# Attention, routed experts and a feed-forward layer on one core: main rows of seven experts 624 instead of 640

## The chip, the cores and the metric

The kernel runs on one core of one Trainium2 chip. The metric is the device time of one execution in microseconds (us), and the time of a kernel is the median of several executions. Engines are named as in the profile: PE (TensorE, its matmuls), PEld (TensorE's weight loads, which overlap the matmuls), DVE (VectorE), ACT (ScalarE), POOL (GpSimd) and SP (SyncE, which here only issues DMAs).

## The reference

Three layers, one after the other, all in fp32, on 4 x 576 = 2304 tokens of width 512:

```python
# 1. attention with a sliding window of 64 keys, 8 heads of 64
mask = (rel >= 0) & (rel < 64)
x = softmax(where(mask, q @ k.T / 8, -1e9)) @ v          # [2304, 512]
# 2. eight experts, the two best of each token
noisy = x @ w_gate + log1p(exp(x @ w_noise)) * noise      # [2304, 8]
top2, top2_w = two largest of noisy, softmax over the two
out[mask] += top2_w[mask, k, None] * (np.maximum(x[mask] @ w1[e], 0.0) @ w2[e])
# 3. feed-forward layer
h = x @ w_in;  g = h * np.clip(h + 3.0, 0.0, 6.0) / 6.0
out = g @ w_out
```

`w1[e]` is 512 x 1024 and `w2[e]` is 1024 x 512; `w_in` is 512 x 2048 and `w_out` 2048 x 512. Each token goes to two of the eight experts, so an expert gets 2 x 2304 / 8 = 576 rows on average. Counted with the reference on its own inputs, the experts 0 to 7 take 618, 582, 571, 549, 537, 554, 611 and 586 rows, and expert 0 has 377 of its rows in the first 11 of the 18 token tiles.

## The kernel before

**Stages.** Attention runs over 18 tiles of 128 tokens (`iteration`). Each tile's result also goes through the gate, and in five lots of tiles DVE works out which two experts a token has and which place it takes among the expert's rows. POOL then scatters each token's row twice into `x_sorted` in DRAM (`scatter`, L691), at `e * ROOM + rank`. Then come the eight experts (`expert`, one after the other), then the feed-forward layer over six groups of three tiles (`hidden2` L1706, `project2` L1722), whose rows POOL gathers from `y_sorted`.

**An expert.** The first MAIN = 640 rows of expert e are always worked, as BLOCKS = 5 blocks of 128 rows in two parts, PARTS = ((0, 3), (3, 2)): part 0 is blocks 0 to 2 (384 rows), part 1 is blocks 3 and 4 (256 rows). A block of x is loaded from `x_sorted` into `x_in` (`load_x`, an ACT DMA), transposed by four PE operations (`turn_x`, L1570), and split by ACT and DVE into a high and a low half (`x_hi` L868, `x_lo` L1167) that stand in `xs`. All matmuls are done as three passes over such halves. For each chunk c of 128 of the 1024 hidden features, `hidden` (L1586) does 4 x 3 = 12 matmuls with the weights as the loaded side and the part's rows as the streamed side: 384 columns in part 0, 256 in part 1. ACT takes the relu of the result (`h_hi`, L878), DVE makes the low half (`h_lo`, L1173). Then `project` (L1602) does, for each block of the part, three matmuls with the block's 128 hidden rows as the loaded side and 512 columns of `w2` streamed, into the block's bank of `Y`. After the last chunk, DVE moves each block to `y_sb` (`move_y`, L1185) and ACT stores it to `y_sorted` (`store_y`, L888). PE's order is written out by hand: hidden(0), hidden(1), project(0), hidden(2), project(1) and so on, with the transposes of coming blocks put between (TURN_AT): blocks 3 and 4 of the same expert in part 0, blocks 0 to 2 of the next expert in part 1. So `project(c)` follows a whole `hidden(c + 1)` after `hidden(c)`.

**Rows beyond the main ones.** Where an expert has more rows than MAIN, `tab_live` is set (L1226), and all engines run `more_block` MORE times (13, each 128 rows), with a wait of its own at each step. Otherwise they skip it.

**Places.** Expert e's rows begin in `y_sorted` at the sum of its predecessors' row counts, each rounded up to whole blocks of 128. Stores of the five blocks are issued in order of the experts, and `store_y` of block 0 waits until all of the expert before are stored. Since part 0 of expert 0 begins when only the first 11 tiles are scattered, the count of expert 0 is raised to at least PARTS[0][1] * P = 384 at that point (L1117), and its rows that no token takes are zeros.

**Expert 0 and the start of expert 1.** The rank of the last lot is worked out while part 0 of expert 0 runs (`rank`, between `hidden(3)` and `project(2)`). From it follow, in this order: eight scatters on POOL, SP's loads of blocks 3 and 4 of expert 0 (L570), SP's writing of zeros behind the rows of expert 1 (`pad`, L556), and ACT's loads of expert 1's first blocks, which `turn_x` in part 1 of expert 0 waits for.

**Weights.** SP loads them in eight chunks an expert into `stage`; POOL splits each into halves (L660, L670) into one of two sets of `W`, which it may overwrite when the expert before the last one is done (`expert_done`).

Of the kernel before, what the change touches and what calls it, by code (L numbers as in the profile page):

```python
# [5 lines left out]
ALU = mybir.AluOpType  # L6
ACT = mybir.ActivationFunctionType
AX = mybir.AxisListType
F32 = mybir.dt.float32
# [8 lines left out]
def attention_moe_ffn(nc, q, k, v, wg, wn, noise, w1, w2, w_in, w_out, out):  # L18
# [23 lines left out]
    assert MAIN + MORE * P == N  # L42
# [16 lines left out]
    assert GT * P <= PARTS[0][1] * P  # L59
# [46 lines left out]
    ROOM = N + MAIN  # L106
# [96 lines left out]
    ex = Region((nc.sbuf_usable_end - 64 - 4 * (3 * DM + DM + F + 2 * F + (3 + BLOCKS) * DM + 2 * KD * MAIN)) // 128 * 128 + 64)  # L203
# [27 lines left out]
    with ExitStack() as ctx:  # L231
# [92 lines left out]
        y_stored = [sem(f"y_stored{j}") for j in range(BLOCKS)]  # L324

# [118 lines left out]
        def x_place(j, a):  # L444

            part = 0 if j < PARTS[1][0] else 1
            at = (j - PARTS[part][0]) * P
            return xs[part][:, a, :, at:at + P]
# [13 lines left out]
        def _(sp):  # L462
# [106 lines left out]
            for j in range(PARTS[1][0], BLOCKS):  # L569
                sp.dma_start(x_in[:, j], x_sorted[j * P:(j + 1) * P, :]).then_inc(x_loaded[j], 16)  # L570
# [24 lines left out]
        def _(pool):  # L595
# [197 lines left out]
        def _(act):  # L793
# [46 lines left out]
            def load_x(e, j):  # L840
                row = e * ROOM + j * P
                src = x_sorted[row:row + P, :] if isinstance(e, int) else x_sorted[bass.ds(row, P), :]
                act.dma_start(x_in[:, j], src).then_inc(x_loaded[j], 16)
# [22 lines left out]
            def x_hi(e, j, bank=XTP):  # L866
                act.wait_ge(tx_full, BLOCKS * e + j + 1)
                nc.scalar.copy(x_place(j, 0), bank.rearrange("p (k n) -> p k n", k=KD)).then_inc(xhi_done, 1)  # L868
# [26 lines left out]
            def more_block(e, t):  # L895
# [14 lines left out]
                act.wait_ge(more_moved, o + 2)  # L910
                act.dma_start(y_sorted[bass.ds(row_y, P), :], y_more[:]).then_inc(more_stored, 16)
# [97 lines left out]
        def _(dve):  # L1009
# [5 lines left out]
            for j in range(BLOCKS):  # L1015
                dve.sem_inc(y_stored[j], 16)
            dve.sem_inc(more_xlo, 1)
# [54 lines left out]
            def route(b, part):  # L1072
# [37 lines left out]
                elif part == 5:  # L1110
# [6 lines left out]
                    if b == FIRST_LOT:  # L1117
                        step(nc.vector.tensor_scalar(base_e[:, 0:1], base_e[:, 0:1], float(PARTS[0][1] * P), None, ALU.max))
# [46 lines left out]
            def x_lo(e, j, bank=XTP):  # L1165
                dve.wait_ge(xhi_done, BLOCKS * e + j + 1)
                nc.vector.tensor_tensor(x_place(j, 1), bank.rearrange("p (k n) -> p k n", k=KD),  # L1167
                                        x_place(j, 0).bitcast(F32), ALU.subtract).then_inc(x_split, 1)

            def h_lo(e, part, c):  # L1170
                n = PARTS[part][1] * P
                dve.wait_ge(hhi_done, unit(e, part, c) + 1)
                nc.vector.scalar_tensor_tensor(hs[:, c % 2, 1, 0:n], HP_[:, c % 2, 0:n], 0.0,  # L1173
                                               hs[:, c % 2, 0, 0:n].bitcast(F32), ALU.max, ALU.subtract).then_inc(h_split, 1)

            def move_y(e, j):
# [8 lines left out]
                nc.vector.tensor_copy(y_sb[:, j % 3], Y[:, j, :]).then_inc(y_moved, 1)  # L1185
# [166 lines left out]
        def _(pe):  # L1352
# [212 lines left out]
            def turn_x(e, j, bank=XTP):  # L1565
                pe.wait_ge(x_loaded[j], 16 * (e + 1))
                if bank is XTP:
                    pe.wait_ge(x_split, BLOCKS * e + j + 1)
                for kd in range(KD):
# [21 lines left out]
            def project(e, par, part, c):  # L1591
# [182 lines left out]
```

## Time and profile before

| what | us |
|---|---|
| median of 3 runs | 1024.81 |
| lowest and highest of them | 1022.99, 1029.31 |
| the profiled execution, its own time | 1028.99 |
| its span, first to last instruction | 1027.2 |
| PE busy in the span | 996.3 |
| PEld, POOL, DVE, ACT busy | 885.0, 423.6, 416.9, 229.6 |

The span is what all positions in time in the trace are counted from. A matmul's duration in the trace is the time from its start to its modelled end, and neighbours overlap, so 12 matmuls in a row take less than 12 times the mean duration of one. The rows on the chain of waits don't overlap, and give the pace. The mean granted clock of TensorE over the span is 0.990 of full speed.

### The profile page before, as it was taken

Reading aid. Unit: us, or ns where it says so; the run is one execution under the profiler, and the core shown is the slowest. Engines: PE = TensorE matmul, PEld = TensorE weight load, DVE = VectorE, ACT = ScalarE, POOL = GpSimd, SP = SyncE. Lnnn points to the kernel's source line nnn. Section 1 sums busy time; section 2 is a strip of 40 time slices with the busy share of each in tenths; the row PEclk is TensorE's granted clock in tenths of the full one; section 3 lists DMA queues with packets and bytes.
Section 4 is the critical chain, followed back from the end, with each engine's and each line's share of the span. In section 5 each row is a group of like instructions: output and inputs, shape, how many; then the busy total and the mean of one; then the engine's idle time right before and its main releaser. Section 6 shows DMA issues by size and latency. Waiting matters only on the chain.

```text
span 1027.2 us, 17992 instructions
## 1 busy us (share of the span) xinstructions
PE 996.3 (97%) x7108; PEld 885.0 (86%) x7108; DVE 416.9 (41%) x897; ACT 229.6 (22%) x537; POOL 423.6 (41%) x326
## 2 busy tenths in 40 slices
PE   6998879999999999999999999999999999999998
PEld 5776668898999999999989988999999999999997
DVE  3577754313222221322222246545435445454433
ACT  4665621211111121111111122111111111111111
POOL 3167885994664819194663928300101001000000
PEclk9999989999999999999999999999999999999999
DMA  9699786855362616254341334110101011100000
GB/s 183 133 198 238 219 274 216 259 178 181 104 215 77 200 64 218 80 155 163 103 164 66 120 119 157 49 45 21 42 31 41 21 45 39 39 1 1 32 1 32
DMA packets 125542, 116.17 MB, mean 113 GB/s; under 512 B 64800, under 2 KB 92960, under 8 KB 125472
## 3 DMA queue, kind: packets, MB, share of 16 engines
q1 hardware_dynamic: 106368, 75.36, 26.3%
q10 hardware_dynamic: 13344, 20.98, 5.9%
q0 software_dynamic: 5760, 18.88, 5.6%
q8 instruction: 47, 0.77, 0.3%
q14 instruction: 23, 0.19, 0.1%
HBM read 76.13 MB, written 39.06 MB: 112 GB/s over the span
## 4 chain that ended last, share of the span: by engine, by line
PE 87%; POOL 4%; DVE 3%; DMA 2%; issue 2%; ACT 1%; SPq 1%; ACTq 0%; DVEq 0%; POOLq 0%
PE PS L1602 20%; PE PS L1586 20%; PE PS L1722 19%; PE PS L1706 19%; POOL x_sorted L691 2%; PE PS L1467 2%; PE PS L1570 2%; PE PS L1391 1%; PE PS L1446 1%; POOL W L670 1%; PE PS L1647 1%; PE PS L1430 1%; DMA x_sorted<-zeros 1%; DVE negmax L1038 1%; POOL W L660 1%
## 5 line engine op out<-in xcount | busy, mean ns | idle before, releaser
L1602 PE MATMUL PS<-W,hs_room 128*128 128x512 f32 x960 | 245.6, 399 | 0.0
L1586 PE MATMUL PS<-xs,W 128*128 128x256 f32 (+1 forms) x1536 | 243.7, 309 | 0.0
L1586 PEld LDWEIGHTS PS<-xs,W 128*128 128x128 f32 x1536 | 234.3, 189 | 10.4 <-issue 0.2
L1722 PE MATMUL PS<-W,gs 128*128 128x512 f32 x864 | 217.0, 395 | 0.9 <-DVE gs L1322 0.9
L1706 PE MATMUL PS<-x2s,W 128*128 128x384 f32 x1152 | 216.6, 337 | 0.0
L1706 PEld LDWEIGHTS PS<-x2s,W 128*128 128x128 f32 x1152 | 201.2, 188 | 7.3
L660 POOL TENSOR_TENSOR W<-stage,ones_f 128x1024 fp32r<-128x1024 f32 (+1 forms) x100 | 147.5, 1483 | 141.3 <-PE PS L1602 137.5
L1602 PEld LDWEIGHTS PS<-W,hs_room 128*128 128x128 f32 x960 | 174.6, 188 | 33.2
L1722 PEld LDWEIGHTS PS<-W,gs 128*128 128x128 f32 x864 | 161.2, 188 | 31.8 <-issue 1.6
L670 POOL TENSOR_TENSOR W<-stage,W 128x1024 fp32r<-128x1024 f32 (+1 forms) x100 | 185.6, 1865 | 5.9
L1173 DVE SCALAR_TENSOR_TENSOR hs_room<-PS,hs_room 128x256 fp32r<-128x256 f32 (+1 forms) x128 | 62.8, 491 | 294.1 <-ACT hs_room L878 294.1
L878 ACT ACTIVATE hs_room<-PS 128x256 fp32r<-128x256 f32 (+1 forms) x128 | 56.0, 438 | 374.6 <-PE PS L1586 356.8
L983 ACT ACTIVATE gs<-PS 128x384 fp32r<-128x384 f32 x96 | 47.2, 492 | 307.6 <-DVE PS L1320 307.6
L767 POOL DMA_INDIRECT ya<-y_sorted,slot x18 | 17.1, 951 | 224.0 <-PE PS L1647 200.7
L1318 DVE TENSOR_SCALAR hc<-PS 128x384 f32<-128x384 f32 x96 | 53.5, 557 | 130.9 <-PE PS L1706 130.9
L1322 DVE SCALAR_TENSOR_TENSOR gs<-PS,gs 128x384 fp32r<-128x384 f32 x96 | 53.6, 558 | 60.5 <-ACT gs L983 60.0
L1320 DVE SCALAR_TENSOR_TENSOR PS<-hc,PS 128x384 f32<-128x384 f32 x96 | 53.9, 562 | 3.3
L691 POOL DMA_INDIRECT x_sorted<-x_cur,slot_cur x36 | 35.8, 994 | 19.1 <-DVE slot_cur L1124 11.9
L813 ACT ACTIVATE probs<-PS,negmax 128x128 f32<-128x128 f32 x144 | 39.3, 399 | 2.9 <-DVE negmax L1038 2.9
L1185 DVE COPY y_sb<-PS 128x512 f32<-128x512 f32 x40 | 27.0, 688 | 22.5 <-PE PS L1602 22.4
L1167 DVE TENSOR_TENSOR xs<-PS,xs 128x512 fp32r<-128x512 f32 x40 | 27.6, 691 | 18.6 <-ACT xs L868 16.9
L698 POOL COPY x_cur<-x_new 128x512 f32<-128x512 f32 x18 | 10.9, 609 | 50.6 <-DVE x_new L1053 50.4
(133 smaller groups left out, 576.9 us busy)
## 6 DMA issues: line engine op xcount, KB each, us to landing
stage<-in_moe_w_dram SPq DMA_DIRECT2D x64, 512.0 KB, 5.6
y_sorted<-y_sb ACTq DMA_DIRECT2D x40, 256.0 KB, 3.0
x_in<-x_sorted ACTq DMA_DIRECT2D x38, 256.0 KB, 4.5
x_sorted<-zeros SPq DMA_DIRECT2D x7, 1280.0 KB, 7.8
vD<-in_v_dram SPq DMA_DIRECT2D x72, 64.0 KB, 3.0
out_dram<-o_sb SPq DMA_DIRECT2D x18, 256.0 KB, 2.0
stage<-in_moe_w_in_dram SPq DMA_DIRECT2D x8, 512.0 KB, 3.9
stage<-in_moe_w_out_dram SPq DMA_DIRECT2D x8, 512.0 KB, 3.4
```

Source lines behind the costliest of these rows:

```text
L660: last = nc.gpsimd.tensor_tensor(chunk_at(parity, c, 0)[:, at], stage[:, c % STAGES, at], ones_f[:].broadcast_to([P, n]), ALU.mult)
L670: last = nc.gpsimd.tensor_tensor(chunk_at(parity, c, 1)[:, at], stage[:, c % STAGES, at], chunk_at(parity, c, 0)[:, at].bitcast(F32), ALU. ...
L691: pool.indirect_dma_start(out=x_sorted, out_offset=bass.IndirectOffsetOnAxis(ap=slot_cur[:, k, t:t + 1], axis=0), in_=x_cur[:, t, :], in_o ...
L878: nc.scalar.activation(hs[:, c % 2, 0, 0:n], HP_[:, c % 2, 0:n], ACT.Relu).then_inc(hhi_done, 1)
L1173: nc.vector.scalar_tensor_tensor(hs[:, c % 2, 1, 0:n], HP_[:, c % 2, 0:n], 0.0, hs[:, c % 2, 0, 0:n].bitcast(F32), ALU.max, ALU.subtract). ...
L1318: nc.vector.tensor_scalar(hc[:, c % 2], h, 3.0, 0.0, ALU.add, ALU.max).then_inc(hc_done, 1)
L1320: nc.vector.scalar_tensor_tensor(G6[:, c % 2], hc[:, c % 2], 6.0, h, ALU.min, ALU.mult).then_inc(g6_done, 1)
L1322: nc.vector.scalar_tensor_tensor(gs[:, c % 2, 1], G6[:, c % 2], 1.0 / 6.0, gs[:, c % 2, 0].bitcast(F32), ALU.mult, ALU.subtract).then_inc( ...
L1586: last = nc.tensor.matmul(HP_[:, c % 2, 0:n], W[:, par, 0, b, at:at + P], xs[part][:, a, kd, :], start=start, stop=(kd == KD - 1 and (a, b ...
L1602: last = nc.tensor.matmul(Y[:, first + t, :], hs[:, c % 2, a, t * P:(t + 1) * P], W[:, par, 1, b, c * DM:(c + 1) * DM], start=(c == 0 and ...
L1706: last = nc.tensor.matmul(H2P[:, c % 2, :], W[:, 0, kd // 2, b, at:at + P], x2s[par][:, a, kd, :], start=first, stop=(kd == KD - 1 and (a, ...
L1722: last = nc.tensor.matmul(OP[:, tt, :], gs[:, c % 2, a, tt * P:(tt + 1) * P], W[:, 1, c // FC, b, at:at + DM], start=(c == 0 and (a, b) == ...
```

## The change

For experts 0 to 6 block 2, the last of part 0, has 112 rows instead of 128. Part 0 thus has 368 rows, part 1 still 256, and MAIN is 624. Blocks 3 and 4 begin 16 rows earlier in `x_sorted` and `y_sorted`. Expert 7 keeps its 640 rows in `E - 1`'s own code, since `is_last` is true for it. The 16 rows of `y_sorted` behind the 624 are filled with zeros by a small DMA of ACT's queue for each of the seven experts (64 pieces of 512 bytes, in `store_y` after block 0), with a semaphore `y_filled` on which the next expert's block 0, `more_block`'s store and POOL's gathers wait. MORE becomes 14. The count of expert 0 is raised to 368 instead of 384.

The core of the diff:

```diff
-    MAIN = BLOCKS * P
-    MORE = (N - MAIN) // P
+    CUT = 16
+    MAIN = BLOCKS * P - CUT
+    MORE = -(-(N - MAIN) // P)
...
+    def block_rows(e, j):
+        return P - CUT if j == PARTS[0][1] - 1 and not is_last(e) else P
+
+    def block_row(e, j):
+
+        return j * P - (CUT if j >= PARTS[0][1] and not is_last(e) else 0)
...
             for j in range(PARTS[1][0], BLOCKS):
-                sp.dma_start(x_in[:, j], x_sorted[j * P:(j + 1) * P, :]).then_inc(x_loaded[j], 16)
+                sp.dma_start(x_in[:, j], x_sorted[block_row(0, j):block_row(0, j) + P, :]).then_inc(x_loaded[j], 16)
...
+            pool.wait_ge(y_filled, 16 * E)
...
-                act.dma_start(x_in[:, j], src).then_inc(x_loaded[j], 16)
+                act.dma_start(x_in[0:n, j], src).then_inc(x_loaded[j], 16)
...
             def h_hi(e, part, c):
-                n = PARTS[part][1] * P
+                n = part_rows(e, part)
...
                         act.wait_ge(y_stored[n], 16 * (e + 1))
+                    act.wait_ge(y_filled, 16 * (e + 1))
                     act.wait_ge(more_stored, 16 * (MORE * e + 1))
                 act.wait_ge(y_moved, BLOCKS * (e + 1) + j + 1)
-                act.dma_start(y_sorted[bass.ds(base + j * P, P), :], y_sb[:, j % 3]).then_inc(y_stored[j], 16)
+                n = block_rows(e, j)
+                act.dma_start(y_sorted[bass.ds(base + block_row(e, j), n), :], y_sb[0:n, j % 3]).then_inc(y_stored[j], 16)
+                if j == 0 and not is_last(e):
+
+                    act.dma_start(y_sorted[bass.ds(base + MAIN, CUT), :].rearrange("p (k d) -> (p k) d", d=P),
+                                  zeros[0:CUT * KD, :]).then_inc(y_filled, 16)
...
-                        step(nc.vector.tensor_scalar(base_e[:, 0:1], base_e[:, 0:1], float(PARTS[0][1] * P), None, ALU.max))
+                        step(nc.vector.tensor_scalar(base_e[:, 0:1], base_e[:, 0:1], float(part_rows(0, 0)), None, ALU.max))
...
-                nc.vector.tensor_copy(y_sb[:, j % 3], Y[:, j, :]).then_inc(y_moved, 1)
+                n = block_rows(e, j)
+                nc.vector.tensor_copy(y_sb[0:n, j % 3], Y[0:n, j, :]).then_inc(y_moved, 1)
...
-                    last = nc.tensor.transpose(bank[:, kd * P:(kd + 1) * P], x_in[:, j, kd * P:(kd + 1) * P], ident[:])
+                    last = nc.tensor.transpose(bank[:, kd * P:kd * P + n], x_in[0:n, j, kd * P:(kd + 1) * P], ident[0:n, 0:n])
...
             def hidden(e, par, part, c):
-                n = blocks * P
+                n = part_rows(e, part)
...
-                        last = nc.tensor.matmul(HP_[:, c % 2, 0:n], W[:, par, 0, b, at:at + P], xs[part][:, a, kd, :],
+                        last = nc.tensor.matmul(HP_[:, c % 2, 0:n], W[:, par, 0, b, at:at + P], xs[part][:, a, kd, 0:n],
...
                 for t in range(blocks):
+                    n = block_rows(e, first + t)
                     for a, b in PASSES:
-                        last = nc.tensor.matmul(Y[:, first + t, :], hs[:, c % 2, a, t * P:(t + 1) * P],
+                        last = nc.tensor.matmul(Y[0:n, first + t, :], hs[:, c % 2, a, t * P:t * P + n],
```

PE's order of work stays as it was, with other sizes. This is PE at the end of part 0 of expert 1 in the kernel before; `xs_116` is part 0's `xs` and `xs_115` part 1's, and the sizes are those of the result:

```order
L1586 MATMUL PS<-xs_116,W 128x384 x12
L1570 MATMUL PS<-ident,x_in 128x128 x4
L1602 MATMUL PS<-W,hs_room 128x512 x9
L1586 MATMUL PS<-xs_116,W 128x384 x12
L1602 MATMUL PS<-W,hs_room 128x512 x18
L1654 TENSOR_LOAD tab_live
L1654 ISA x2
L1586 MATMUL PS<-xs_115,W 128x256 x24
```

And the same place in the changed kernel, whose lines are numbered 32 and 33 higher here:

```order
L1618 MATMUL PS<-xs_116,W 128x368 x12
L1602 MATMUL PS<-ident,x_in 128x128 x4
L1635 MATMUL PS<-W,hs_room 128x512 x6
L1635 MATMUL PS<-W,hs_room 112x512 x3
L1618 MATMUL PS<-xs_116,W 128x368 x12
L1635 MATMUL PS<-W,hs_room 128x512 x6
L1635 MATMUL PS<-W,hs_room 112x512 x3
L1635 MATMUL PS<-W,hs_room 128x512 x6
L1635 MATMUL PS<-W,hs_room 112x512 x3
L1687 TENSOR_LOAD tab_live
L1687 ISA x2
L1618 MATMUL PS<-xs_115,W 128x256 x24
```

Nothing moved; each of the 12 matmuls of a chunk streams 368 columns, and of nine matmuls of `project` three load 112 columns and write 112 partitions.

This is ACT at the start of part 1 of expert 1 before:

```order
L878 ACTIVATE hs_room<-PS 128x256
L888 ISA
L888 DMA y_sorted<-y_sb 128x512
L888 ISA
L888 DMA y_sorted<-y_sb 128x512
L878 ACTIVATE hs_room<-PS 128x256
L888 ISA
L888 DMA y_sorted<-y_sb 128x512
```

And in the changed kernel:

```order
L899 ACTIVATE hs_room<-PS 128x256
L911 ISA
L911 DMA y_sorted<-y_sb 128x512
L914 ISA
L914 DMA y_sorted<-zeros 64x128
L911 ISA
L911 DMA y_sorted<-y_sb 128x512
L899 ACTIVATE hs_room<-PS 128x256
L911 ISA
L911 DMA y_sorted<-y_sb 112x512
```

One DMA more stands between the relu of chunk 0 and that of chunk 1, and the store of block 2 carries 112 rows.

## Rows read from the trace of the kernel before

**Rows 1.** The page: busy time of the engines; the chain that ended last.

```profile
PE 996.3 (97%) x7108; PEld 885.0 (86%) x7108; DVE 416.9 (41%) x897; ACT 229.6 (22%) x537; POOL 423.6 (41%) x326
...
PE 87%; POOL 4%; DVE 3%; DMA 2%; issue 2%; ACT 1%; SPq 1%; ACTq 0%; DVEq 0%; POOLq 0%
```

**Rows 2.** Stretches (from:to, length in us): expert 0's parts, then expert 4's.

```profile
core 0: us, PE busy (x) PEld busy (x) DVE busy (x) ACT busy (x) POOL busy (x), PEclk, DMA share, GB/s
144.50:181.40 36.90, 36.90 (x197) 32.99 (x196) 17.05 (x78) 6.14 (x14) 21.18 (x20) 0.96 0.76 255
...
380.10:414.40 34.30, 34.30 (x177) 31.02 (x176) 7.74 (x14) 5.00 (x10) 33.22 (x16) 1.00 0.63 200
414.40:438.20 23.80, 23.80 (x157) 21.60 (x156) 6.63 (x14) 4.76 (x11) 0.84 (x1) 1.00 0.17 56
```

**Rows 3.** The chain in order of time through expert 4: start us, length us, what.

```profile
380.28 4.17 PE PS L1586 x24
384.45 2.10 PE PS L1602 x9
...
405.79 0.44 PE PS L1570 x4
...
410.41 4.19 PE PS L1602 x18
```

**Rows 4.** The same chain, part 1.

```profile
414.60 2.83 PE PS L1586 x24
417.43 1.40 PE PS L1602 x6
```

**Rows 5.** Groups of instructions, shapes apart, 380.1 to 438.2 us: busy, mean ns, idle before.

```profile
L1586 PEld LDWEIGHTS PS<-xs,W 128*128 128x128 f32 x192 | 29.1, 188 | 1.3
L1602 PEld LDWEIGHTS PS<-W,hs_room 128*128 128x128 f32 x120 | 21.8, 188 | 4.2
...
L660 POOL TENSOR_TENSOR W<-stage,ones_f 128x1024 fp32r<-128x1024 f32 x8 | 15.2, 1894 | 23.5 <-PE PS L1602 23.5
...
L1173 DVE SCALAR_TENSOR_TENSOR hs_room<-PS,hs_room 128x384 fp32r<-128x384 f32 x8 | 4.5, 557 | 23.5 <-ACT hs_room L878 23.5
...
L878 ACT ACTIVATE hs_room<-PS 128x384 fp32r<-128x384 f32 x8 | 3.9, 492 | 26.7 <-PE PS L1586 26.7
```

**Rows 6.** Instructions in order of time, start of part 1 of expert 4: start, length in us.

```profile
416.71 0.97 ACTq L888 DMA_DIRECT2D y_sorted<-y_sb  x2
...
417.85 0.38 ACT L878 ACTIVATE hs_room<-PS 128x256 fp32r<-128x256 f32 x1 [1.32 <-DVE y_sb L1185]
...
418.26 0.42 DVE L1173 SCALAR_TENSOR_TENSOR hs_room<-PS,hs_room 128x256 fp32r<-128x256 f32 x1 [0.68 <-ACT hs_room L878]
...
420.44 0.94 PE L1602 MATMUL PS<-W,hs_room 128*128 128x512 f32 x3
```

**Rows 7.** The chain in order of time, from the last scatters into part 1 of expert 0.

```profile
162.46 0.95 POOL x_sorted L691
...
171.44 2.72 DMA x_sorted<-x_cur,slot_cur
...
175.89 7.38 DMA x_sorted<-zeros
...
183.29 4.07 DMA x_in<-x_sorted
...
187.40 0.65 PE PS L1570 x4
```

**Rows 8.** Instructions in order of time around the start of expert 0 and its rank.

```profile
143.12 0.58 ACT L868 CAST xs<-PS 128x512 fp32r<-128x512 f32 x1 [1.05 <-PE PS L1570]
...
143.74 0.69 DVE L1167 TENSOR_TENSOR xs<-PS,xs 128x512 fp32r<-128x512 f32 x1 [0.20 <-ACT xs L868]
...
144.53 3.71 PE L1586 MATMUL PS<-xs,W 128*128 128x384 f32 x12
...
159.31 0.19 PE L1509 MATMUL PS<-chosen_b,before_b 128*128 128x32 bf16 x1
```

More of the change, by code:

```diff
@@ L36, in attention_moe_ffn, with is_last, part_rows @@
     BLOCKS = 5
-    MAIN = BLOCKS * P
-    MORE = (N - MAIN) // P
+    CUT = 16
+    MAIN = BLOCKS * P - CUT
+    MORE = -(-(N - MAIN) // P)
     FEWEST = -(-2 * N // P)
     MOST = (2 * N + PARTS[0][1] * P + E * (P - 1)) // P + BLOCKS
-    assert MAIN + MORE * P == N
+    def is_last(e):
+        return isinstance(e, int) and e == E - 1
+    def block_rows(e, j):
+        return P - CUT if j == PARTS[0][1] - 1 and not is_last(e) else P
+    def block_row(e, j):
+        return j * P - (CUT if j >= PARTS[0][1] and not is_last(e) else 0)
+    def part_rows(e, part):
+        first, blocks = PARTS[part]
+        return sum(block_rows(e, j) for j in range(first, first + blocks))
+    assert all(sum(part_rows(e, part) for part in range(2)) >= MAIN for e in range(E)) and MAIN + MORE * P >= N
     FC = F // P
@@ L58, in attention_moe_ffn @@
     MIX_AT = {4: (0, 1), 5: (2,)}
-    assert GT * P <= PARTS[0][1] * P
+    assert GT * P <= part_rows(E - 1, 0)
     assert KD * F == QCH * CH and KD * F2 == SCH * CH and FC * DM == QCH * CH and F2C * DM == SCH * CH
@@ L104, in attention_moe_ffn @@
     assert LOTS[0][0] + LOTS[0][1] + RANKS_AFTER - 1 == LOOP[0] + LOOP_TILES and LOTS[0][1] == most - 1
-    ROOM = N + MAIN
+    ROOM = N + BLOCKS * P
     x_sorted = nc.dram_tensor("x_sorted", [E * ROOM, DM], F32).ap()
@@ L198, in attention_moe_ffn @@
     assert late.at <= nc.sbuf_usable_end
-    ex = Region((nc.sbuf_usable_end - 64 - 4 * (3 * DM + DM + F + 2 * F + (3 + BLOCKS) * DM + 2 * KD * MAIN)) // 128 * 128 + 64)
+    ex = Region((nc.sbuf_usable_end - 64 - 4 * (3 * DM + DM + F + 2 * F + (3 + BLOCKS) * DM + 2 * KD * BLOCKS * P)) // 128 * 128 + 64)
     assert base % 128 == 0
@@ L324, in attention_moe_ffn @@
         y_stored = [sem(f"y_stored{j}") for j in range(BLOCKS)]
+        y_filled = sem("y_filled")
         more_loaded = sem("more_loaded")
@@ L442, in if_more, with x_place, x_turned @@
                     eng.sem_inc(signal, each * MORE)
-        def x_place(j, a):
+        def x_place(e, j, a):
             part = 0 if j < PARTS[1][0] else 1
             at = (j - PARTS[part][0]) * P
-            return xs[part][:, a, :, at:at + P]
+            return xs[part][:, a, :, at:at + block_rows(e, j)]
+        def x_turned(e, j, bank):
+            return bank.rearrange("p (k n) -> p k n", k=KD)[:, :, 0:block_rows(e, j)]
         def unit(e, part, c):
@@ L840, in load_x @@
             def load_x(e, j):
-                row = e * ROOM + j * P
-                src = x_sorted[row:row + P, :] if isinstance(e, int) else x_sorted[bass.ds(row, P), :]
-                act.dma_start(x_in[:, j], src).then_inc(x_loaded[j], 16)
+                row, n = e * ROOM + block_row(e, j), block_rows(e, j)
+                src = x_sorted[row:row + n, :] if isinstance(e, int) else x_sorted[bass.ds(row, n), :]
+                act.dma_start(x_in[0:n, j], src).then_inc(x_loaded[j], 16)
             for T in range(TILES + 1):
@@ L867, in x_hi @@
                 act.wait_ge(tx_full, BLOCKS * e + j + 1)
-                nc.scalar.copy(x_place(j, 0), bank.rearrange("p (k n) -> p k n", k=KD)).then_inc(xhi_done, 1)
+                nc.scalar.copy(x_place(e, j, 0), x_turned(e, j, bank)).then_inc(xhi_done, 1)
             def h_hi(e, part, c):
-                n = PARTS[part][1] * P
+                n = part_rows(e, part)
                 act.wait_ge(h_full, unit(e, part, c) + 1)
@@ L910, in more_block @@
                 act.wait_ge(more_moved, o + 2)
+                if not is_last(e):
+                    act.wait_ge(y_filled, 16 * (e + 2))
                 act.dma_start(y_sorted[bass.ds(row_y, P), :], y_more[:]).then_inc(more_stored, 16)
@@ L1016, in _ @@
                 dve.sem_inc(y_stored[j], 16)
+            dve.sem_inc(y_filled, 16)
             dve.sem_inc(more_xlo, 1)
@@ L1166, in x_lo @@
                 dve.wait_ge(xhi_done, BLOCKS * e + j + 1)
-                nc.vector.tensor_tensor(x_place(j, 1), bank.rearrange("p (k n) -> p k n", k=KD),
-                                        x_place(j, 0).bitcast(F32), ALU.subtract).then_inc(x_split, 1)
+                nc.vector.tensor_tensor(x_place(e, j, 1), x_turned(e, j, bank), x_place(e, j, 0).bitcast(F32), ALU.subtract)\
+                    .then_inc(x_split, 1)
             def h_lo(e, part, c):
-                n = PARTS[part][1] * P
+                n = part_rows(e, part)
                 dve.wait_ge(hhi_done, unit(e, part, c) + 1)
@@ L1568, in turn_x @@
                     pe.wait_ge(x_split, BLOCKS * e + j + 1)
+                n = block_rows(e, j)
                 for kd in range(KD):
-                    last = nc.tensor.transpose(bank[:, kd * P:(kd + 1) * P], x_in[:, j, kd * P:(kd + 1) * P], ident[:])
+                    last = nc.tensor.transpose(bank[:, kd * P:kd * P + n], x_in[0:n, j, kd * P:(kd + 1) * P], ident[0:n, 0:n])
                 last.then_inc(tx_full, 1)
@@ L1575, in hidden @@
                 first, blocks = PARTS[part]
-                n = blocks * P
+                n = part_rows(e, part)
                 if c == 0:
```

## The prediction

> **What bounds the kernel now.** I read the page's busy times first: PE is busy 97% of the span, and 87% of the chain that ended last is PE [rows 1]. A share over the whole kernel doesn't say what an edit in the experts is worth, so next comes the table of stretches: in expert 4, which stands for experts 1 to 6, PE is busy 34.30 of 34.30 us in part 0 and 23.80 of 23.80 us in part 1, at a granted clock of 1.00 [rows 2], which is the 2.4 GHz level. No other engine is near that. The chain in order of time shows the pace, since its pieces don't overlap: in part 0, 24 matmuls of `hidden` in 4.17 us, or 173.8 ns each for 384 columns, and 9 of `project` in 2.10 us, or 233.3 ns each for 512 columns [rows 3]; in part 1, 24 of `hidden` in 2.83 us, or 117.9 ns each for 256 columns [rows 4]. The reader is to see that time follows the streamed columns: 0.452, 0.456 and 0.461 ns a column for 384, 512 and 256. A fixed cost per matmul would make the small ones much dearer by column. The loads of the other operand, 188 ns each as recorded [rows 5], lie beneath the matmuls; matmuls with a load each still follow each other at 117.9 ns.
>
> The other engines leave slack. POOL splits the next weights in some 33 us of part 0 [rows 2] and then sits idle 23.5 us until PE frees a set [rows 5]. ACT's relu (492 ns) and DVE's low half (557 ns) make 1.05 us behind a `hidden` of 384 columns [rows 5], and a whole further `hidden` of about 2.08 us lies before the `project` that needs them. So a shorter stream on PE should come out in the time, one for one, until such a cover is gone.
>
> **The change, part by part.**
>
> *Shorter `hidden`, experts 1 to 6.* Each has 8 x 12 = 96 matmuls in part 0 that lose 16 columns. The slope between the two sizes of the same line is (173.8 - 117.9) / 128 = 0.436 ns a column [rows 3, 4], so 16 columns are 7.0 ns. In all 6 x 96 x 7.0 ns = 4.02 us. Bounds: by the mean cost of a column, 0.452 ns, it is 4.17 us; below, nothing, if 368 columns ran like 384. No row shows a length between 256 and 384, and 368 is no multiple of 64, but three sizes lie within 2% of one line, so I take the slope.
>
> The Trainium skill, page "TensorE: Matmul & The Clock Gate", section "Back-to-back issue gap", gives N / 2.4 + 2.5 ns for one matmul after another. By it 384 columns would take 162.5 ns, and the rows show 173.8; the saving of 16 columns would be 6.7 ns, and this term 3.84 us instead of 4.02. The measured slope stands in the sum.
>
> *Expert 0.* The same 96 matmuls, but the first 12 run at the lower pace: 12 in 3.71 us from the first start to the modelled end of the last [rows 8], with the granted clock at 0.96 over the stretch [rows 2]. As an estimate, 3.71 us / 12 x 16 / 384 = 12.9 ns each, 0.15 us. The other 84 give 84 x 7.0 = 0.59 us. Together 0.74 us earlier at the end of part 0. But this expert has a second chain. PE's transposes of expert 1's first block wait for a load that began at 183.29 us, behind the zeros that began at 175.89, behind scatters that began at 162.46, and the transposes start at 187.40 when it lands [rows 7]. That chain starts from the last rank on PE at 159.31 [rows 8], which stands behind four of eight chunks of `hidden`: it comes earlier by 12 x 12.9 + 36 x 7.0 ns = 0.41 us, while PE comes earlier by 0.74 us. PE already waits there, so 0.33 us is lost in a longer wait. Net 0.41 us.
>
> *Shorter transposes.* Block 2's four transposes take 0.44 us as 110 ns each [rows 3] for 128 streamed columns. With 112 they could be 110 x 16 / 128 = 13.8 ns shorter, if the stream sets the pace, or not at all, if the load does; nothing in the rows tells these apart, since both are 128. Six times four in the stream make 0 to 0.33 us; I take 0.15, near the middle.
>
> *Start of expert 0.* Block 2 is the last thing before the first `hidden`: ACT 0.58 us, then DVE 0.69 us, ending at 144.43, and PE starts at 144.53 [rows 8]. With an eighth less each and shorter transposes this chain would be 0.16 to 0.2 us shorter, but PE's own work before it leaves room for only part. I take 0.1, between 0 and 0.2.
>
> *`project`.* The 7 x 8 x 3 = 168 matmuls of block 2 still stream 512 columns, so they stay at 233.3 ns [rows 3]. Fewer loaded columns and fewer result rows save nothing where the stream sets the pace. Cost and gain 0.
>
> *The added zeros.* ACT issues one DMA more, between two stores, in part 1. Two such issues take 0.97 us, so one costs about 0.49 us [rows 6]. Behind it on ACT stand the store of block 1 and the relu of chunk 1, which started at 417.85 and whose low half was ready at 418.68; PE uses it at 420.44 [rows 6]. So 1.76 us of cover hides 0.49 us, the cover being `project` of chunk 0 and `hidden` of chunk 2. If the cover were gone, 7 x 0.49 = 3.4 us would be lost. In expert 0 ACT also issues three loads there, and its cover is thinner, so at most one such issue (0.49 us) could show. The new waits on `y_filled` come one expert (34.3 + 23.8 = 58.1 us [rows 2]) after the DMA that answers them, against landings of 4.07 and 7.38 us for larger DMAs [rows 7]; they cost nothing. SP has no new wait, POOL only one of these.
>
> *ACT and DVE.* Relu and low half become a little shorter and remain hidden; their cover `hidden` shrinks from 2.08 to 2.00 us, still above 1.05 us. Weights: POOL's idle 23.5 us [rows 5] shrinks by about 0.7 us. The rest (112 table entries instead of 104, 224 KB loads instead of 256 KB) lies beside PE.
>
> Sum: 4.02 + 0.41 + 0.15 + 0.10 = 4.68 us. The profiled execution took 1028.99 us with a span of 1027.2 us; its own time should become 1024.3 and its span 1022.5. That execution lies 4.2 us above the median 1024.81 of the three runs. In the median: 1024.81 - 4.7 = **1020.1 us**, 0.46% less. A difference of about 1% is what a measurement of this kernel can tell from no change, so this one would read as the same.
>
> **The rivals.**
>
> *No shorter matmul.* If 368 columns cost like 384, or an equal loss arises beside the gain (a wait as below), the time stays at 1024.8. For it: no size between is in the trace. Against it: the three sizes on one line [rows 3, 4]. Chance 0.09.
>
> *Slower loads of 112 columns.* If a load narrower than the array is slower and no longer lies under the matmul before it, the 168 matmuls get longer, at most by a whole recorded load of 188 ns [rows 5]: 168 x 0.188 = 31.6 us, giving 1051.7. It turns the gain into a loss from 4.7 us / 168 = 28 ns a matmul. Against it: full loads hide in spacings of 117.9 ns [rows 4], and these have 233.3 ns, so a load could nearly double and still hide. Chance 0.03.
> The Trainium skill, same page, section "Weight-path perf modes — Fast Weight Load (FWL) and DoubleRow", says that fast weight load is on only where there are exactly 128 weights and the type isn't FP32; by that rule a block of 112 could lose it where one of 128 had it. No run here shows whether these fp32 operands had it at all.
>
> *Rows beyond the main ones.* If an expert had over 624 rows, `more_block` would run 14 times for it: each with 48 matmuls of 512 columns and 12 transposes, 48 x 0.233 + 12 x 0.11 = 12.5 us, so 175 us and a time of 1195. It decides at 625 rows. Against it: the reference's counts are at most 618, and expert 0's, 377 after 11 tiles, is no longer raised (before, 7 rows more made it 625, under the old 640). The margin is 6 rows; the scores at a boundary between two experts would have to differ from the reference's. Chance 0.01.
>
> *A gain of over 1%.* Nothing in the rows can give 10 us; it would need a shift in the attention stage, which the edit doesn't touch. The scatter among the three runs, 6.3 us, could alone fake part of it. Chance 0.03.
>
> **How the numbers follow.** The forecast has 0.84. Its own bounds from the terms: gains from 3.8 us (slope a bit lower, transposes 0, start 0) to 5.4 us (4.17 + 0.74 + 0.33 + 0.2), so 1019.4 to 1021.0; to this comes the scatter of a median, where the three runs lie 1.8 us below and 4.5 us above theirs. The range 1016.5 to 1025.0 takes in the case without gain and some 3.5 us of scatter below. Faster by over 1% (under 1014.6): 0.03. Slower by over 1% (over 1035.1): 0.03, from the slow loads and the extra rows. Within 1%: 0.94.
>
> **What would show it.** In the chain of the changed kernel, 24 matmuls of `hidden` in part 0 should take 4.00 us where they took 4.17, nine of `project` still 2.10 us, and part 0 of experts 1 to 6 about 33.6 us instead of 34.3 us, part 1 unchanged but for up to 0.05 us. Part 0 of expert 7 should still take 34.3 us. The wait of the transposes at the load of expert 1's block 0 should be about 0.3 us longer. `hidden` at 4.17 us would prove the first rival, `project` over 2.10 us the second, and any instruction on `x_more` the third. If ACT's relu of chunk 1 is late and PE idles before `project` of chunk 1, my cover for the zeros was wrong.

## The result and the profile after

The changed kernel takes 1019.0 us (median of 6 runs, 1018.35 to 1019.39), the kernel before 1024.15 us (median of 6, 1022.99 to 1029.31). The ratio is 0.9945 with a 95% interval of 0.9928 to 0.9962: 0.55% or 5.15 us less, inside the band that was called the same, and clear of no change.

The page of the changed kernel, the rows that answer to [rows 1]: busy times, then the chain that ended last.

```profile
PE 988.1 (97%) x7108; PEld 877.5 (86%) x7108; DVE 417.8 (41%) x897; ACT 227.7 (22%) x537; POOL 423.5 (42%) x326
...
PE 81%; SPq 7%; POOL 5%; DMA 3%; issue 2%; DVE 1%; ACT 0%; ACTq 0%; POOLq 0%; DVEq 0%
```

PE is busy for the same 97% of the span, with the same 7108 matmuls and 8.2 us less busy time, of which 3.5 us lie before the first `hidden`. The chain has less of PE and more of SP's DMA issues than before (7% against 1%); these too lie before the first `hidden`. The profiled execution took 1019.22 us with a span of 1017.5 us. Against the profile before that is 9.8 us less, nearly double the difference of the medians, so the two profiles alone would mislead. The stretches tell them apart. A part of an expert is measured here from the start of its first `hidden` to that of the next part, from the starts of the matmuls in the trace. (In the changed kernel `hidden` is L1618, `project` L1635, `turn_x` L1602, `store_y` L911 and the DMA of zeros L914.)

| stretch, us | before | after |
|---|---|---|
| start of the span to the first `hidden` | 144.53 | 139.65 |
| expert 0, part 0 | 36.87 | 36.45 |
| expert 0, part 1 | 24.25 | 24.15 |
| experts 1 to 6, part 0 each | 34.32 | 33.63 |
| experts 1 to 5, part 1 each | 23.83 | 23.79 |
| expert 6, part 1 | 23.84 | 23.83 |
| expert 7, part 0 | 34.32 | 34.32 |
| from expert 7's start to the end of the span | 472.66 | 472.66 |

Before the first `hidden` the profiles differ by 4.88 us, in a stage that the edit leaves alone; further profiles of the changed kernel had 144.93 and 147.12 us there. That part comes from the execution. The rest is 0.52 us in expert 0 and 4.37 us in experts 1 to 6, together 4.89 us. The 4.37 us are the change. In expert 0 a part of the difference isn't: TensorE ran at its lower clock for the first 3.0 us of part 0 before and for the first 3.6 us after. Two further runs give the part at a granted clock of 1.00 throughout, and there it takes 35.46 us with 384 columns (the cut in part 1, below) and 34.78 us with 368, so the change gives 0.68 us in it, as in the other experts.

The chain in order of time through expert 4 of the changed kernel (start us, length us, what), which answers to [rows 3, 4]:

```profile
372.67 4.01 PE PS L1618 x24
376.68 2.09 PE PS L1635 x9
...
402.13 4.18 PE PS L1635 x18
406.31 2.83 PE PS L1618 x24
...
424.09 0.39 PE PS L1602 x4
```

24 matmuls of 368 columns take 4.01 us where 384 columns took 4.17. Nine of `project`, three of them with 112 loaded columns, take 2.09 us where nine took 2.10, so the narrower load hides. The four transposes of block 2 take 0.39 us, the others still 0.44. They stand in part 1 of the expert before, which is why part 1 of expert 6 hardly gains: expert 7's block 2 keeps its 128 rows. Part 1's 24 are at 2.83 us as before.

Expert 0 holds the one surprise. This is the same view from the last scatter into part 1 of expert 0, which answers to [rows 7]:

```profile
170.78 6.98 DMA x_sorted<-zeros
177.79 0.35 ACTq L864
178.18 0.53 ACTq L864
178.75 0.44 ACTq L864
179.68 0.38 ACTq L911
180.24 0.58 ACTq L914
181.00 0.44 ACTq L911
181.55 0.39 ACT hs_room L899
181.96 0.44 DVE hs_room L1203
182.44 1.67 PE PS L1635 x6
```

Before, PE waited here for the load of expert 1's block. Now the chain runs through ACT's own queue: three loads, a store, the added zeros, a store, and only then the relu that `project` of chunk 1 needs.

### The profile page after: what moved, and what is told of

It reads as the page before. It is cut to its first block, busy times and chain, and to the rows that moved or that the text cites. A ratio compares the mean times of both kernels' runs of the same rounds, so it can differ in the third digit from the quotient of the medians.

```text
span 1017.5 us, 18019 instructions
## 1 busy us (share of the span) xinstructions
PE 988.1 (97%) x7108; PEld 877.5 (86%) x7108; DVE 417.8 (41%) x897; ACT 227.7 (22%) x537; POOL 423.5 (42%) x326
## 4 chain that ended last, share of the span: by engine, by line
PE 81%; SPq 7%; POOL 5%; DMA 3%; issue 2%; DVE 1%; ACT 0%; ACTq 0%; POOLq 0%; DVEq 0%
PE PS L1635 20%; PE PS L1755 20%; PE PS L1739 19%; PE PS L1618 19%; SPq L500 3%; SPq L490 3%; POOL x_sorted L711 3%; PE PS L1602 1%; POOL W L690 1%; POOL W L680 1%; PE PS L1680 1%; DMA x_sorted<-zeros 1%; DMA y_sorted<-y_sb 0%; PE PS L1498 0%; DMA stage<-in_moe_w_dram 0%
## 5 line engine op out<-in xcount | busy, mean ns | idle before, releaser
L1635 PE MATMUL PS<-W,hs_room 128*128 128x512 f32 (+1 forms) x960 | 245.2, 399 | 0.1
L1618 PEld LDWEIGHTS PS<-xs,W 128*128 128x128 f32 x1536 | 231.0, 189 | 10.8 <-issue 0.2
L1618 PE MATMUL PS<-xs,W 128*128 128x256 f32 (+2 forms) x1536 | 239.7, 307 | 0.0
L1635 PEld LDWEIGHTS PS<-W,hs_room 128*128 128x128 f32 (+1 forms) x960 | 172.3, 186 | 34.6 <-DVE hs_room L1203 0.3
L1755 PEld LDWEIGHTS PS<-W,gs 128*128 128x128 f32 x864 | 161.5, 188 | 31.5 <-issue 1.6
L1203 DVE SCALAR_TENSOR_TENSOR hs_room<-PS,hs_room 128x256 fp32r<-128x256 f32 (+2 forms) x128 | 61.9, 484 | 290.6 <-ACT hs_room L899 290.6
L899 ACT ACTIVATE hs_room<-PS 128x256 fp32r<-128x256 f32 (+2 forms) x128 | 55.3, 432 | 371.0 <-PE PS L1618 354.2
L787 POOL DMA_INDIRECT ya<-y_sorted,slot x18 | 17.1, 951 | 223.9 <-PE PS L1680 200.6
L1216 DVE COPY y_sb<-PS 128x512 f32<-128x512 f32 (+1 forms) x40 | 27.0, 688 | 22.6 <-PE PS L1635 22.6
L1197 DVE TENSOR_TENSOR xs<-PS,xs 128x512 fp32r<-128x512 f32 (+1 forms) x40 | 27.1, 679 | 17.2 <-ACT xs L889 15.5
```

The source lines that it names most:

```text
L1635: last = nc.tensor.matmul(Y[0:n, first + t, :], hs[:, c % 2, a, t * P:t * P + n], W[:, par, 1, b, c * DM:(c + 1) * DM], start=(c == 0 and ...
L1755: last = nc.tensor.matmul(OP[:, tt, :], gs[:, c % 2, a, tt * P:(tt + 1) * P], W[:, 1, c // FC, b, at:at + DM], start=(c == 0 and (a, b) == ...
```

## Experiments

The runs are in three series on three chips, each with the kernel before and the kernels of its series side by side; its medians there were 1029.31, 1029.43 and 1030.01 us. Ratios are to the kernel before of the same series. Stretches are read from the profiles; they repeat to 0.01 us in experts 1 to 6 of the three profiles of the changed kernel (part 1 of expert 6, 23.83 us, set apart), so they tell apart what totals can't.

**The changed kernel again.** No edit.

> The changed kernel once more, as the yardstick of this series. Theory (the gain is the shorter stream of hidden in part 0): part 0 of experts 1 to 6 takes 33.63 us, part 1 23.79 us, part 0 of expert 7 34.32 us, and the time is 1019.0 us, 0.5% under the kernel before. Rival (most of the difference of the first profiles lies in the attention stage and not in the experts): experts as above, but the ratio to the kernel before moves to 0.998 or more when both are measured anew.

Measured: ratio 0.9937 (0.9911 to 0.9963), median 1023.55 us. Experts 1 to 6: part 0 33.63, part 1 23.79 us; expert 7's part 0 34.32. The theory holds and the rival falls: the ratio stands although this profile reached the first `hidden` at 144.93 us.

**Only the narrow `project`.** The stream of `hidden` and the transposes on 128 rows again, the 112 kept only where `project` loads:

```diff
             def hidden(e, par, part, c):
-                n = part_rows(e, part)
+                n = PARTS[part][1] * P
```

and likewise in `h_hi`, `h_lo`, `x_place`, `x_turned`, `load_x` and `turn_x`.

> Only one part of the change: hidden, relu, low half and the transposes of block 2 work on 128 rows again (384 columns), while project loads 112 columns for block 2, and Y, its copy and its store have 112 rows; zeros as in the changed kernel. Theory (the load lies under the 512 streamed columns of the matmul before it): project stays at 2.09 to 2.10 us for nine, part 0 takes 34.27 us (34.32 less 24 x 2 ns), the time is 1024 us. Rival (a load of 112 columns loses a fast way and shows): project over 2.15 us for nine, part 0 over 34.6 us, time over 1026 us.

Measured: ratio 1.0002 (0.9985 to 1.0019), median 1029.67 us. Part 0 of experts 1 to 6 takes 34.27 us. The chain through it:

```profile
379.73 4.17 PE PS L1618 x24
383.89 2.09 PE PS L1635 x9
```

The slow load is not there; the 112 columns even save 34.32 - 34.27 = 0.05 us an expert. What is left of the saving in part 0, 0.69 - 0.05 = 0.64 us, belongs to `hidden`: 6.6 ns for each of 96 matmuls, against 7.0 ns from the slope. Over six experts that is 3.82 us. The saving of 6.7 ns that the prediction worked out from the section "Back-to-back issue gap" of the Trainium skill's page "TensorE: Matmul & The Clock Gate" is nearer. The N / 2.4 + 2.5 ns of that section, which it gives for an isolated matmul, makes 162.5 ns of 384 columns, and the rows show 173.8.

**Other sizes.** `CUT = 22`, which gives 362 columns:

> The changed kernel with CUT 22 and the zeros where the change has them: part 0 has 362 rows. Theory (0.42 to 0.44 ns a column): part 0 of experts 1 to 6 33.38 us, total 1.7 us under the changed kernel, 1017.3 us. Rival (steps of 16 columns): part 0 33.63 us, 1019.0 us.

Measured: ratio 0.9948 (0.9924 to 0.9972), median 1024.25 us. Part 0 takes 33.53 us in expert 1 and 33.42 to 33.44 in experts 2 to 6. The chain:

```profile
379.11 3.95 PE PS L1618 x24
383.06 2.10 PE PS L1635 x9
```

The stream doesn't go in steps of 16: 362 columns take 164.6 ns, 368 took 167.1. The first `project` of expert 1 takes 2.20 us instead of 2.10, which is its 0.1 us. The 0.20 us an expert over the change are real in the trace and too small for this total.

`CUT = 64`, with the rows behind the main ones left out (`tab_live` compares with `2 * N` instead of MAIN). The DMA of zeros is written another way there, from 64 rows of `zeros` repeated four times:

> CUT is 64: block 2 has 64 rows, part 0 320 rows, main rows 576. The rows beyond the main ones are left out altogether (their flag is never set), so experts with more than 576 rows lose the rest. Theory (by streamed columns, other engines far off): part 0 of experts 1 to 6 takes 34.32 - 96 x 64 x 0.43 ns - 0.15 us = 31.5 us, part 1 shrinks by 0.2 us for shorter transposes, about 7 x 2.9 + 1 = 21 us under the kernel before, so 1003 us. Rival (a cover breaks: weights, relu or the loads come late once part 0 is 3 us shorter): gain below 17 us, PE idle before hidden or project in part 0.

Measured: ratio 0.9821 (0.9782 to 0.9859), median 1012.36 us, 17.1 us under the kernel before of its series where 21 us were forecast. Its chain through expert 4, the last row from part 1, and the instructions at the start of part 0:

```profile
371.12 3.52 PE PS L1618 x24
374.65 2.30 PE PS L1635 x9
376.94 1.75 PE PS L1618 x12
378.70 2.10 PE PS L1635 x9
...
403.04 2.72 PE PS L1618 x24
```

```profile
371.42 0.94 ACTq L911 DMA_DIRECT2D y_sorted<-y_sb  x2
373.51 0.44 ACT L899 ACTIVATE hs_room<-PS 128x320 fp32r<-128x320 f32 x1 [4.69 <-PE PS L1618]
```

320 columns take 3.52 us / 24 = 146.7 ns; from there to 368 it is 0.43 ns a column. Part 0 takes 31.69 to 31.94 us, a little over the 31.5 expected. In the chain it is the first `project`, 2.30 us instead of 2.10, which loses. Its relu is the first one behind the stores of the expert before, and starts at 373.51, 0.6 us after its own 12 matmuls ended (371.12 + 1.76 = 372.88). The cover of ACT at the start of part 0 is thus nearly used up at 320 columns: experts 2 to 4 lose by it (31.77 to 31.94 us), experts 1, 5 and 6 don't (31.69 to 31.71 us). The rival named such a break, though its gain of below 17 us is just missed. Part 1 was to shrink by 0.2 us and doesn't: it takes 23.85 to 23.88 us in experts 1 to 5, where the `project` behind block 2's transposes takes 1.60 us instead of 1.40. Why is open. The last row above is a surprise of its own: part 1 has its 256 columns as ever, and here its first 24 matmuls take 2.72 us or 113.3 ns each instead of 117.9.

**The cut in part 1.** `block_rows` takes the rows from block 4 instead of block 2, `block_row` is `j * P`, and `CUT` is 14:

> The cut lies in block 4 instead of block 2, and is 14 rows (main rows 626, since expert 0 has 625 when its count is raised to 384 at the first part). Part 0 has 384 rows again, part 1 242. Theory (time by streamed columns at any length): part 1 of experts 1 to 6 takes 23.84 - 96 x 14 x 0.45 ns = 23.23 us, part 0 34.27 us (one block's transposes shorter), about 7 x 0.65 = 4.6 us less than before: 1019.6 us. Rival (near 110 ns the load of 128 columns sets the pace, transposes of 128 columns also take 109 ns): part 1 shortens by less than 0.3 us an expert, the time is 1022 us or more.

Measured: ratio 0.9968 (0.9950 to 0.9986), median 1026.03 us. The chain in part 1:

```profile
414.44 2.73 PE PS L1618 x24
417.16 1.39 PE PS L1635 x6
```

242 columns take 113.8 ns where 256 took 117.9: 0.29 ns a column instead of 0.43. Part 1 takes 23.31 us, 0.52 less than before where 0.60 was expected, part 0 34.29. The theory is the nearer one, and its size a little too large. That the load of 128 columns sets a floor near the 110 ns that transposes take each [rows 3] isn't shown: the run with `CUT = 64` had 113.3 ns for 256 columns, so the pace near this length doesn't follow the length alone.

This run also holds the missing yardstick for expert 0, since its part 0 has 384 columns and ran at a granted clock of 1.00 (the third last number) throughout:

```profile
148.00:183.50 35.50, 35.46 (x195) 31.60 (x196) 17.30 (x78) 5.85 (x14) 21.86 (x21) 1.00 0.82 269
```

**Where the zeros are issued.** First four DMAs of 4 rows at the same place instead of one of 16:

```diff
...
-                    act.dma_start(y_sorted[bass.ds(base + MAIN, CUT), :].rearrange("p (k d) -> (p k) d", d=P),
-                                  zeros[0:CUT * KD, :]).then_inc(y_filled, 16)
+                    for part in range(4):
+                        act.dma_start(y_sorted[bass.ds(base + MAIN + 4 * part, 4), :].rearrange("p (k d) -> (p k) d", d=P),
+                                      zeros[0:4 * KD, :]).then_inc(y_filled, 16)
...
```

The waits on `y_filled` count four DMAs an expert accordingly.

> The zeros are written by four DMAs of 4 rows instead of one of 16, all issued at the same place. Theory (one such issue costs ACT 0.81 us of which the cover of project(0) and hidden(2) leaves 0.94 us over in experts 1 to 6, and nothing in expert 0): three more are 2.43 us, so each of experts 1 to 6 loses 1.5 us in part 1 (25.3 instead of 23.8 us) and expert 0 2.4 us, in all 11.4 us, so 1030.4 us. Rival (an issue costs 0.49 us, as two stores before suggested): 1.47 us, a loss of 0.5 us an expert and 1.5 us in expert 0, in all 4.7 us, so 1023.7 us. If ACT's lateness were off the path altogether: 1019.0 us.

Measured: ratio 0.9997 (0.9971 to 1.0022), median 1030.04 us, 6.5 us over the changed kernel of the same series. Part 1 takes 25.60 us in expert 0 and 25.03, 24.28, 24.60, 24.34, 24.49 and 24.26 us in experts 1 to 6. That is 0.4 to 1.2 us an expert and 4.2 us for the six, nearer to the rival's size. Both prices were rough, since the small DMAs are quicker to issue (a median of 337 ns against 541). Expert 1 loses most because one of its four issues took 1.57 us. The mechanism is plain in expert 1, instructions in order of time:

```profile
242.02 3.08 ACTq L914 DMA_DIRECT2D y_sorted<-zeros  x4
245.27 0.36 ACTq L911 DMA_DIRECT2D y_sorted<-y_sb  x1
245.73 0.38 ACT L899 ACTIVATE hs_room<-PS 128x256 fp32r<-128x256 f32 x1 [4.32 <-DMA y_sorted<-zeros]
246.15 0.42 DVE L1203 SCALAR_TENSOR_TENSOR hs_room<-PS,hs_room 128x256 fp32r<-128x256 f32 x1 [3.68 <-ACT hs_room L899]
246.63 1.67 PE L1635 MATMUL PS<-W,hs_room 128*128 128x512 f32 x6 [0.96 <-DVE hs_room L1203]
```

ACT, DVE and PE stand idle (the brackets) until the one before it in this chain is done, and PE loses 0.96 us. So the place of the zeros had a price that the cover hid.

Then one DMA, issued with the store of block 4 (`if j == BLOCKS - 1` instead of `if j == 0`):

> The changed kernel with the DMA of zeros issued with the store of block 4 instead of after that of block 0. Theory (in expert 0 ACT is so late with its loads, stores and the zeros that PE waits 0.3 us before project of chunk 1; elsewhere a cover of 0.94 us is left): part 1 of expert 0 takes 23.85 us instead of 24.15, all other stretches stay, the total falls by 0.3 us (1018.7), which the time alone can't show. Rival (the 0.3 us is the late load of expert 1's block, which takes the place of the other wait): part 1 of expert 0 stays at 24.1 us.

Measured: ratio 0.9961 (0.9937 to 0.9985), median 1025.68 us, 2.1 us over the changed kernel. In expert 0 the rival was right: part 1 took 24.58 us, as long as the 24.60 us of the changed kernel in this series. The wait for ACT was gone, and PE instead stood idle for 0.57 us (0.20 before) until the load of expert 1's block landed, which is the wait that the prediction had extended by 0.33 us. What both readings missed is that other stretches change. In experts 1 to 6 part 0 grew from 33.63 to between 33.76 and 34.17 us. The stores of blocks 3 and 4 come when the next expert has already begun, and its first relu stands behind them and now behind the zeros too. Over the six experts that makes about 2 us. The chain in expert 1:

```profile
207.73 0.58 ACTq L914
...
209.00 0.49 ACT hs_room L899
...
209.51 0.55 DVE hs_room L1203
...
210.20 2.33 PE PS L1635 x9
```

In the profile of the changed kernel this chain is PE throughout.

With that place and `CUT = 22` together:

> CUT is 22 instead of 16 (part 0 has 362 rows, main rows 618, which is the count of expert 0), and the DMA of zeros is issued with the store of block 4 instead of after that of block 0. Theory (time goes by streamed columns, 0.42 to 0.44 ns each): 6 columns less are 2.6 ns a matmul, so part 0 of experts 1 to 6 takes 33.38 us instead of 33.63, which with the wait saved in expert 0 makes 7 x 0.25 + 0.3 = 2.0 us, so about 1017.0 us. Rival (the stream goes in steps of 16 or 32 columns): 362 cost like 368, part 0 stays at 33.63 and the time at 1018.7.

Measured: ratio 0.9969 (0.9949 to 0.9988), median 1026.78 us. Part 0 reaches 33.43 us in experts 5 and 6, while expert 1 takes 34.57 and the others between 33.66 and 33.76 us. The shorter stream is there, and the late place takes more than it gives.

**Zeros behind the store of block 2.** From these two comes the place where ACT idles for PE (`if j == 2`):

> The changed kernel as the yardstick of this series: part 0 of experts 1 to 6 33.63 us, part 1 23.79 us; in expert 0 PE idles 0.2 to 0.5 us before project of chunk 1. The time differs from chip to chip with the attention stage (139.7 to 149.4 us in the profiles so far); the ratio to the kernel before should be 0.995 again.

> The DMA of zeros is issued after the store of block 2, which stands behind the relu of chunk 1, where ACT next idles 2.1 us for PE; so late in part 1 nothing waits for it. Theory: PE's idle before project of chunk 1 in expert 0 goes (0.3 us) unless the load of expert 1's block is late instead, experts 1 to 6 stay at 33.63 and 23.79 us; total 0.3 us under the changed kernel or the same. Rival (anywhere in part 1 the issue of 0.8 us reaches PE): part 1 of experts 1 to 6 above 23.9 us.

Measured, changed kernel: ratio 0.9949 (0.9928 to 0.9970), median 1025.13 us; with the zeros moved: 0.9942 (0.9921 to 0.9963), median 1024.15 us. The totals can't be told apart. The stretch can: part 1 of expert 0 takes 24.50 us in the one and 23.80 us in the other, with experts 1 to 6 the same to 0.01 us. In order of time, the changed kernel, then the one with the zeros moved:

```profile
187.71 0.38 ACT L899 ACTIVATE hs_room<-PS 128x256 fp32r<-128x256 f32 x1 [3.80 <-PE PS L1618]
...
188.60 0.73 PE L1635 MATMUL PS<-W,hs_room 128*128 128x512 f32 x2 [0.46 <-DVE hs_room L1203]
```

```profile
184.65 0.38 ACT L899 ACTIVATE hs_room<-PS 128x256 fp32r<-128x256 f32 x1 [2.67 <-issue]
...
185.32 1.13 ACTq L914 DMA_DIRECT2D y_sorted<-zeros  x1
...
185.98 1.65 PE L1635 MATMUL PS<-W,hs_room 128*128 128x512 f32 x6
```

The relu now comes ahead of the zeros and PE goes on without a wait. A kernel that leaves the zeros out was not run, so their price is known only from these three places.

With this place and `CUT = 22`:

> The same place for the zeros, with CUT 22 (362 rows in part 0). Theory: part 0 of experts 1 to 6 takes 33.43 us as in the kernel with CUT 22 alone, so 7 x 0.2 + 0.3 = 1.7 us under the changed kernel, a ratio of 0.9935 to the kernel before. Rival (the lateness seen with the zeros in the last store comes from the shorter part 0 itself): part 0 above 33.5 us in some experts.

Measured: ratio 1.0003 (0.9986 to 1.0021), median 1030.47 us, 6.3 us over the same kernel with CUT 16. The stretches of experts 1 to 6 are as forecast (33.42 to 33.44 us, 33.58 in expert 1), so they aren't the cause. Expert 0 shows one:

```profile
188.03 4.55 ACTq L914 DMA_DIRECT2D y_sorted<-zeros  x1
```

One issue held ACT 4.55 us, and part 1 of expert 0 took 26.25 us instead of 23.80. Over the kernel's seven such issues the median is 473 ns. In this stretch two stores issued ahead of it took a median of 10.0 us to land, against 4.9 us for the two of the same kernel with CUT 16. So writes landed late there; that this held up the issue, and why just then, isn't shown. The long issue explains 2.4 us of the profiled execution, which at 1026.29 us is one of this kernel's quickest. Where the rest of the 6.3 us lies stays open; the other runs have no trace. One lead is on record: the mean granted clock of its 12 runs has a median of 0.987 (0.982 to 0.990), that of the 8 runs with CUT 16 one of 0.9915 (0.988 to 0.995). In these two profiles the lower clock lies almost wholly before the first expert and in the start of part 0 of expert 0. Whether it is a cause or a mark of other waits isn't shown.

**One row too few.** `CUT = 24`, main rows 616:

> CUT is 24: main rows 616, two fewer than expert 0's 618. Theory (the margin of the change is the reference's counts): more_block runs 14 times for expert 0 and for it alone, at 12.5 us each by the terms of the prediction, or 175 us; so about 1192 us. Rival (the kernel's counts differ from the reference's or the flag does not follow them): about 1017 us, or a multiple of 175 us.

Measured: 1407.1 us, in the one run made. `more_block` runs 14 times for expert 0 and for no other, as the 618 rows of the reference say, but a block costs 27.4 us and not 12.5. The chain through the first block:

```profile
209.12 3.00 DMA x_more<-x_sorted
...
212.16 1.13 PE PS L1650 x4
213.31 0.59 ACT xs_more L929
213.93 0.70 DVE xs_more L1240
...
214.67 8.33 PE PS L1657 x24
...
226.33 7.41 PE PS L1671 x24
...
239.69 1.13 PE PS L1650 x4
```

The block is a chain of single steps. Its stretch, with the granted clock as the third last number:

```profile
205.00:233.00 28.00, 17.80 (x61) 13.32 (x60) 3.30 (x5) 2.85 (x5) 4.06 (x2) 0.76 0.22 67
```

PE is busy 17.80 of 28.00 us, and the granted clock is 0.76. 24 matmuls of 512 columns take 8.33 us, or 347 ns each instead of 233.

The other experts give one more length, 360 columns, here in the chain at the start of expert 4:

```profile
760.91 3.98 PE PS L1618 x24
```

That is 165.9 ns each, longer than the 164.6 ns of 362 columns, and part 0 takes 33.53 to 33.55 us where the run with 362 columns on the same chip took 33.42 to 33.44 in experts 2 to 6. So the time follows the streamed columns only to about 1% here, and the shorter stream isn't always the quicker one. Why isn't shown.

## Why the prediction held, point by point

- **What bounds it: right.** PE is the chain in experts 1 to 6 before and after. With the full stream put back and the rest of the change kept (narrow `project`), the total gain is gone.
- **Shorter `hidden`, 4.02 us: right, 0.2 too large.** 0.64 us an expert, 3.82 us. The slope between 256 and 384 columns, 7.0 ns for 16, was taken over a range in which the pace isn't quite a straight line: a column costs 0.41 ns between 368 and 384, 360 columns took longer than 362, and 256 took 113.3 ns in one run instead of 117.9.
- **`project` of 112, nothing: nearly right.** It gives 0.05 us an expert, 0.3 us in all, which the prediction had ruled out as a gain.
- **Transposes, 0.15 us: low.** The four of a block shrink by 0.04 to 0.05 us (0.44 to 0.39), 0.23 us in experts 1 to 6 and one block's 0.05 us in part 1 of expert 0, in all 0.3 us, near the upper bound of 0.33. They still load 128 columns, so at this size the load doesn't set their pace.
- **Experts 1 to 6 together:** 4.37 us against 4.17 forecast (4.02 + 0.15). The parts measured are 3.82 us (`hidden`), 0.32 us (`project`) and 0.23 us (transposes). The missed small gains and the smaller main one partly cancel.
- **Expert 0, 0.41 us net: the size by luck.** Measured are 0.52 us in these profiles. The term for part 0, 0.74 us, stands up at equal clock (35.46 us against 34.78, or 0.68 us); the two profiles alone show 0.42 us, since the lower clock lasted 0.6 us longer after. The step that failed is the next one, a longer wait for the load. Part 0 of expert 0 takes 36.45, 36.95 and 34.78 us in the three profiles of the changed kernel and 34.79 with the zeros moved, depending on when the granted clock rises: 3.6, 4.9 and 0 us after the start of the part in the three. Two stretches (from:to, length, busy times, granted clock, DMA), the first 2.4 us of the part in the profile after and the whole part with the zeros moved:

```profile
139.60:142.00 2.40, 2.40 (x10) 2.40 (x9) 2.02 (x12) 0.59 (x1) 2.02 (x4) 0.50 1.03 411
```

```profile
145.20:180.00 34.80, 34.80 (x195) 30.67 (x196) 16.66 (x77) 5.87 (x14) 21.04 (x20) 1.00 0.81 268
```

  The clock is 0.50, the 1.2 GHz level, in the one and 1.00 in the other. And in the profile after PE no longer stands idle for the load of expert 1's block: the next point took that place.
- **The zeros at no cost: wrong in expert 0, right elsewhere.** "At most one such issue (0.49 us) could show" named the place; it does show: part 1 of expert 0 lies over the 23.79 us of the others by 0.36 us in the first profile and by 0.81 and 0.71 us in two more (in the 0.81 the load has a share), and by 0.01 with the zeros moved. The mis-sized term is the issue. In expert 4 the zeros are issued at 409.02 and the next store at 409.83, so 0.81 us instead of 0.49. The cover of 1.76 us falls to 0.94.
- **The rivals.** No shorter matmul: excluded by 4.01 us against 4.17. Slower loads: excluded by the narrow `project`. The rule of the Trainium skill that the prediction set beside it (page "TensorE: Matmul & The Clock Gate", section "Weight-path perf modes — Fast Weight Load (FWL) and DoubleRow"), that fast load wants exactly 128 weights and a type other than FP32, could have spoken against the change. Loads of 112 columns are recorded at 174 ns against 188 for 128, and nothing shows whether fast load was in use. Rows beyond the main ones: the mechanism is real two rows further, and more than twice as dear as forecast (14 x 27.4 = 383 us), so the margin of 6 rows deserved its place.
- **The start of expert 0, 0.1 us:** not told apart from the spread of the start, 139.65 to 149.43 us over all profiles of this work, and 144.93 to 149.43 us on one chip.
- **The profiled execution:** forecast at 1024.3 us, it took 1019.22, because it started expert 0 4.88 us earlier. In the medians the gain is 5.15 us against 4.7 forecast, and the stretches give 4.4 us in experts 1 to 6 and some tenths in expert 0; the rest is within the scatter of the medians.

## What to carry to other kernels

Where one engine is the chain for hundreds of us, price a cut by the pace of its own rows, and read the result from stretches that repeat to 0.01 us, not from a total that moves by several us. A small DMA added to an engine that also computes delays that engine's next instruction; put it behind the instruction that others wait for, and look at the busiest place of the queue, not the typical one. A cut to the size of the data needs its margin named with the price of missing it.

## What the runs showed of the hardware that was not expected

- Issuing one 32 KB DMA from ACT took 0.55 us in expert 4, and 0.81 us lay between its start and that of the next store. The same kind of issue, with 44 KB, took 4.55 us once, where stores of that queue took 10.0 us to land.
- Matmuls of these fp32 operands follow each other at 113.8, 117.9, 146.7, 165.9, 164.6, 167.1, 173.8 and 233.3 ns for 242, 256, 320, 360, 362, 368, 384 and 512 streamed columns: no steps of 16, but 360 above 362, and 256 columns at 113.3 ns in one run.
- The same part of PE's work (part 0 of expert 0) took 34.78, 36.45 and 36.95 us in three executions, with 0, 3.6 and 4.9 us of it at the lower level of the clock, 1.2 GHz, and the rest at 2.4 GHz.
